# Three places of an instruction order in a fused attention and two-layer feed-forward kernel: low parts of a, loads of tokens ahead of stores, and parts of weight sums

## The reference

```python
scores = scale * np.matmul(q, k.transpose(0, 1, 3, 2))
out    = np.matmul(scores * Dmat, v)              # Dmat: gamma_h ** (i - j), causal
x      = tokens(out)                              # 2304 x 512
xn     = x / sqrt(mean(x * x) + 1e-6) * rms_g
g      = xn @ w_gate                              # 512 x 1536
y      = (g * sigmoid(g) * (xn @ w_val)) @ w_out  # 1536 x 512
h      = y @ w_in                                 # 512 x 2048
gh     = where(h >= 1, h, where(h <= -1, 0, (h + 1) ** 2 / 4))
result = gh @ w_out2                              # 2048 x 512
```

## Time and profile before

| | |
|---|---|
| median of three runs | 904.11 us (901.4 to 905.42) |
| the profiled execution | 900.61 us, of which the span of instructions is 898.8 us |
| TensorE busy | 870.4 us, 97% of the span |
| VectorE busy | 571.9 us, 64% |
| ScalarE busy | 464.2 us, 52% |
| GpSimd busy | 251.9 us, 28% |
| granted TensorE clock, mean | 0.998 of full speed |
| DMA | 124.09 MB, mean 138 GB/s |

### The profile page before, as it was taken

One profiled execution on the slowest core, in us unless ns is written; L12 is line 12 of the kernel. 1 busy time (PEld: TensorE's weight loads), 2 busy tenths in 40 slices (PEclk: granted clock), 3 DMA queues, 4 the chain that ended last, 5 costly groups with the idle time before them and its releaser, 6 DMA issues.

```text
span 898.8 us, 17947 instructions
## 1 busy us (share of the span) xinstructions
PE 870.4 (97%) x7448; PEld 848.8 (94%) x7448; DVE 571.9 (64%) x799; ACT 464.2 (52%) x732; POOL 251.9 (28%) x172
## 2 busy tenths in 40 slices
PE   6898999999999999999999998999999999999998
PEld 5787999999999999999999988999999978999998
DVE  3599866477953653622242577766567879888884
ACT  2556654445654555511231457877778846433331
POOL 0236763446764664000040422404042000000000
PEclk9999999999999999999999999999999999999999
DMA  9984132333336336334633134233326673444442
GB/s 259 234 248 142 54 104 91 101 100 100 101 100 240 101 100 211 133 106 134 207 103 132 54 132 152 106 128 126 132 112 217 200 237 118 119 140 118 140 119 71
DMA packets 113329, 124.09 MB, mean 138 GB/s; under 512 B 6784, under 2 KB 85760, under 8 KB 113248
## 3 DMA queue, kind: packets, MB, share of 16 engines
q1 hardware_dynamic: 113248, 122.95, 43.5%
HBM read 80.45 MB, written 42.47 MB: 137 GB/s over the span
## 4 chain that ended last, share of the span: by engine, by line
PE 79%; DVE 7%; DMA 5%; ACT 3%; issue 2%; POOL 2%; SPq 1%; DVEq 0%; ACTq 0%
PE pair L727 14%; PE pair L729 14%; PE pair L728 14%; PE pair L825 6%; PE pair L827 6%; PE pair L826 6%; PE pair L888 5%; PE pair L890 5%; PE pair L889 5%; DMA a_kt<-ktok 4%; PE pair L858 1%; DVE cb L1496 1%; PE pair L859 1%; PE pair L860 1%; DVE wq L1528 1%
## 5 line engine op out<-in xcount | busy, mean ns | idle before, releaser
L727 PE MATMUL pair<-xc,wc 128*128 128x288 f32 x672 | 199.4, 297 | 0.6 <-ACT cp L1014 0.4
L728 PE MATMUL pair<-xc,wc 128*128 128x288 f32 x672 | 198.2, 295 | 0.0
L729 PE MATMUL pair<-xc,wc 128*128 128x288 f32 x672 | 197.6, 294 | 0.0
L1014 ACT ACTIVATE cp<-pair 128x576 f32<-128x576 f32 x160 | 103.4, 647 | 156.3 <-PE pair L729 150.2
L1679 POOL TENSOR_TENSOR wc<-wt,wc 128x512 fp32r<-128x512 f32 x84 | 122.6, 1483 | 92.2 <-ACT wc L947 86.6
L727 PE MATMUL pair<-xc,wr 128*128 128x288 f32 x448 | 133.6, 298 | 6.8 <-ACT cp L1014 6.3
L728 PE MATMUL pair<-xc,wr 128*128 128x288 f32 x448 | 132.2, 295 | 0.0
L729 PE MATMUL pair<-xc,wr 128*128 128x288 f32 x448 | 131.7, 294 | 0.0
L727 PEld LDWEIGHTS pair<-xc,wc 128*128 128x128 f32 x672 | 125.9, 187 | 1.6 <-issue 1.5
L729 PEld LDWEIGHTS pair<-xc,wc 128*128 128x128 f32 x672 | 126.6, 188 | 0.0
L728 PEld LDWEIGHTS pair<-xc,wc 128*128 128x128 f32 x672 | 126.2, 188 | 0.0
(11 more groups left out here) (124 smaller groups left out, 1702.6 us busy)
## 6 DMA issues: line engine op xcount, KB each, us to landing
b_scratch<-cb SPq DMA_DIRECT2D x32, 576.0 KB, 2.9
a_scratch<-cb SPq DMA_DIRECT2D x24, 576.0 KB, 2.9
av_r<-a_scratch SPq DMA_DIRECT2D x8, 1728.0 KB, 8.3
wt<-wB SPq DMA_DIRECT2D x72, 128.0 KB, 2.9
bt<-b_scratch SPq DMA_DIRECT2D x28, 256.0 KB, 2.8
bt<-b_scratch SPq DMA_DIRECT2D x56, 128.0 KB, 3.0
a_k<-kT SPq DMA_DIRECT2D x16, 288.0 KB, 8.0
a_q<-qT SPq DMA_DIRECT2D x16, 288.0 KB, 6.8
```

Of the source, the lines that this page charges most:

```text
L727: pe.matmul(o, wh, xh, start=FIRST[i] and j == 0, stop=False, skip_group_check=True)
L728: pe.matmul(o, wh, xl, start=False, stop=False, skip_group_check=True)
L729: mm = pe.matmul(o, wl, xh, start=False, stop=j == 1, skip_group_check=True)
L1014: act.activation(copied(g, n)[:, :, :], pair[(X, Q, X, X)[n]][:, :, 0:HALF], ACT.Copy).then_inc(s_c, 1)
```

## The change

Three things change places; no instruction is added or taken away, and no buffer changes.

- VectorE, last step of stage 2: two of the four low parts of the first half tile of `a` come ahead of `c22_c21` of that step, two stay behind it.
- SP: `load_b(3)` and `load_b(4)` come ahead of the two stores of the last step of stage 4, each with its own wait on `s_q`.
- ScalarE and VectorE: high and low parts of the weight sums of r = 1 and r = 2 are made behind the parts of tokens 4 and 5, so among the plain quarters. Those of r = 3 are made one place earlier: on VectorE at k = 9 in place of those of r = 2, on ScalarE ahead of `b_hi(10)`.

```diff
@@ SyncE
-            store_b(GALL - 1, 0)
             sp.wait_ge(s_q, 2)
             load_b(3)
-            store_b(GALL - 1, 1)
+            store_b(GALL - 1, 0)
             sp.wait_ge(s_q, 4)
             load_b(4)
+            store_b(GALL - 1, 1)
@@ ScalarE
             plain_b_hi(4)
+            sum_w_hi(1)
             plain_b_hi(5)
+            sum_w_hi(2)
             plain_w_hi(3, range(4))
             plain_b_hi(6)
             plain_b_hi(7)
             b_hi(8)
-            sum_w_hi(1)
             plain_out(0)
             b_hi(9)
             plain_out(1)
-            sum_w_hi(2)
...
-                b_hi(k)
                 if k == 10:
                     sum_w_hi(3)
+                b_hi(k)
@@ VectorE, stage 2
+                if g == GB - 1:
+                    a_lo(0, 0)
+                    a_lo(0, 1)
                 c22_c21(g)
...
-                if g == GB - 1:
-                    for c in range(4):
-                        a_lo(0, c)
+            a_lo(0, 2)
+            a_lo(0, 3)
             gated(GB - 1)
@@ VectorE, stage 5
             plain_b_lo(4)
+            sum_w_lo(1)
             plain_b_lo(5)
+            sum_w_lo(2)
             wq_sums(3)
             plain_w_lo(3)
             plain_b_lo(6)
...
                 if k == 8:
-                    sum_w_lo(1)
                     plain_out(0)
                 if k == 9:
                     plain_out(1)
-                    sum_w_lo(2)
-                if k == 10:
                     sum_w_lo(3)
```

## The result

The changed kernel ran in 900.53 us (median of 12 runs, 897.66 to 904.73), the kernel before in 904.63 us beside it (12 runs, 901.4 to 907.97). The ratio is 0.9954 with a 95% interval of 0.9935 to 0.9973: -4.1 us, between -2.4 and -5.9. The forecast was 901.8 (899.3 to 904.8), a gain of 2.3.

What follows compares the result with a forecast made beforehand. TensorE, busy nearly all the time at 2.4 GHz, was taken as the bound, so only its stops could be gained. -2.1 + 0.9 - 0.15 - 0.9 = -2.25, so -2.3: 904.11 to 901.8 us, range 899.3 to 904.8.

Steps and rivals of the forecast that it cites:

- Term 1: Ahead of stage 3: TensorE's stop for the first low part of `a` goes, -2.1 us.
- Terms 2 to 4: Stage 5: new stop at quarter 6, +0.9 us; shorter stop at quarter 9, -0.15; no stop at quarter 10, -0.9.
- tokens in time: Rival, stage 5: tokens 5 arrive by 729.7, quarter 6 does not stop; -3.9, 900.2 us; chance 0.12.
- given back in stage 4: Rival: stage 4's first steps keep their time, the gain ahead of stage 3 is lost; -0.2, 903.9 us; chance 0.08.
- Tokens 5 were not later: Rival, stage 5: tokens 5 arrive late, sharing the rings with `load_b(8)`; quarter 6 later, +1.1, 905.2 us; chance 0.05.
- Quarter 10's stop: Rival, stage 5: moving the weight sums leaves this stop in place; -1.4, 902.7 us; no chance of its own given.

Runs made afterwards that it cites:

- e5_b5_first: Changed kernel with load_b(5) issued ahead of load_wq(3), with its own wait for quarter 2; ratio 0.9934 (0.9902 to 0.9967) against the kernel before.

## Why the prediction was right

**Term 1** (-2.1) measured -2.1 from stage 2 to quarter 0, and -2.06 for the stop. Each step of the order on VectorE came within 0.1 us of what was worked out.

**Terms 2 to 4.** Quarter 0 to quarter 8 took 754.10 - 708.64 = 45.46 us in place of 44.54: +0.92, forecast +0.9. Two small errors cancel in it. Eight quarters without a stop take 43.6 us; the forecast had 43.8, since its 5.475 us a quarter is an average that takes in the quarter behind a stop (5.56, the others 5.44 to 5.46). And the stop at quarter 6 was 1.76 rather than 1.6, with 0.1 more behind it. Quarter 8 to the end took 1.0 less (145.4 against 146.4), forecast 1.05. The stop at quarter 9 stayed with 1.07, that at quarter 10 went. Tokens 5 came 1.48 us earlier, forecast 1.5, by counting the bytes ahead of them. A match to 0.02 is luck: over the seven profiles with the old order on SP they come 24.9 to 25.5 us behind the start of quarter 0, over the six with the changed order (e5_b5_first, which loads tokens 5 earlier still, left out) 23.1 to 23.9. The means, 25.1 and 23.5, are 1.6 apart. The two experiments that change the chain or the arrival alone gave D within 0.2 us of that arithmetic. The -2.2 of D against a forecast of -2.3 is therefore no accident.

**What the forecast lacked** is the price of a stop beyond its length. I costed the 2.07 us at 2.07. The runs show that in three of five profiles the clock was granted at half behind it, 1.5 us more. By these counts the change removes 3/5 x 1.5 = 0.9 us more, and brings some of it back at quarter 6 (one of its three profiles, 1.6 us, so 0.5): -2.2 - 0.9 + 0.5 = -2.6 us on average. The mean D of three profiles each is 536.5 before and 534.2 after, -2.3. Timed, the change measured -4.1 (-2.4 to -5.9) and, again, -3.3 (-1.2 to -5.1).

The clock of the timed runs says where the rest lies. Among runs with the same mean granted clock the changed kernel was 2.9 us faster at 0.994, 2.5 at 0.996 and 2.1 at 0.998; with a straight line through all 24 and 88 runs the difference at equal clock is 2.6 us, give or take 0.7, which holds the -2.2 of the stops. The higher mean clock of the changed kernel, 0.9965 against 0.9954, is worth another 0.9 us, give or take 0.8. Together that is the 3.5 us by which the means of all these runs differ. So the forecast had the stops right and put the clock at nothing; of the first measurement's 4.1 us some 0.6 is left, inside its interval. The runs come from several batches, and those of the kernel before that were timed beside the first measurement have no clock on record, so the split is an estimate from the others. In the batch of the changed kernel's second measurement alone the mean clocks hardly differ (0.9959 and 0.9956), and it was 3.3 us faster there all the same.

Luck has a part in the time as such. By the prediction's own cases 900.2 us is what tokens in time would have given, and the measured 900.53 us lies nearer to that than to the forecast 901.8. Only the profile, with its stop at quarter 6, tells the two apart.

Single profiles scatter in the stages ahead, which D leaves out: stage 2 started between 88.0 and 94.2 us in these fourteen profiles, more than all that is in question. Ten of the fourteen had a lowered clock in the attention stage for 3 to 10 us; they started stage 2 at 91.3 on average, the other four at 89.0 (88.0 to 90.3), so the clock is a part of that scatter but not the whole. Nothing in the profiles says that the change could move it.

**The rivals.** Tokens 5 in time did not happen: quarter 6 stopped for 1.76 us. Term 1 was not given back in stage 4: the distance to stage 4 fell in full, and from the first matmul of stage 4 to quarter 0 it is 189.1 us in all fourteen profiles. Tokens 5 were not later. Quarter 10's stop did go.

## What to carry to other kernels

When a piece of work is moved into an engine's idle time, follow the chain behind it to the next deadline: the same 2.41 us were free between tokens 4 and 5 and cost a stop between tokens 5 and 6, and a slot further on they were free again. Each of these places can be read from start times and one count of bytes ahead in the queue, to some 0.5 us, since that is how far a load's arrival scattered here. And when only a per cent is at stake, compare profiles piece by piece from a common instruction; whole spans here differed by 0.7 us in the wrong direction while the part behind the changed place had gained 2.2.

## What the runs showed of the hardware

Behind a stop of TensorE of about 2 us the granted clock was 0.5 (1.2 GHz in place of 2.4) for some 3 us in three of five profiles of the same 2.07 us stop ahead of stage 3, and in one of four behind stops of 1.5 to 2.2 us at quarter 6. Behind 4.66 us it was lowered (one profile, and ten timed runs with a mean clock of 0.9922 against 0.9954), behind 1.16 us it was not (one profile). A lowered clock cost 1.5 us behind the 2.07 us stop, 1.6 at quarter 6 and 1.9 behind 4.66. Behind the stop of 1.84 to 1.86 us early in stage 4 it was lowered in none of fourteen profiles, so the length of a stop alone does not decide. What does, and why the same stop has two outcomes, is open; it was not tried.
